# A filter and expert kernel: half of the third batch brought back in column tiles, the second batch's way back drawn into the last 24-point stage

## What is computed

```
out[i] = gate_w[i] * (relu(x[i] @ w1[e]) @ w2[e])
```

## Time and profile before

| what | value |
|---|---|
| runs | 571.74, 576.24, 576.70 us (median 576.24) |
| the profiled execution | 571.98 us, of which the span from the first to the last instruction is 570.1 us |
| mean granted TensorE clock | 0.944 of full speed |
| busy share of the span | TensorE 85%, weight loads 68%, VectorE 39%, ScalarE 37%, GpSimd 38% |
| moved by DMA | 121.22 MB, 213 GB/s over the span |

### The profile page before, as it was taken

How to read it: one execution, slowest core, us unless ns; L and a number is a source line. 1 busy time by engine, 2 the same in 40 slices (tenths; PEclk the granted TensorE clock), 3 DMA queues, 4 the chain that set the end, 5 groups by cost and what they waited for, 6 DMA issues and landing times.

```text
span 570.1 us, 9642 instructions
## 1 busy us (share of the span) xinstructions
PE 483.7 (85%) x3864; PEld 386.9 (68%) x3864; DVE 220.1 (39%) x334; ACT 213.7 (37%) x378; POOL 216.8 (38%) x189
## 2 busy tenths in 40 slices
PE   5457676899989958977981699999999999999995
PEld 2124232355545534667971699999999999999994
DVE  6024132233355769167700453324433244332210
ACT  2202222444525535635110445424454244443320
POOL 7070100000000000484077227765587655876212
PEclk9859998999989988899986799999999999999999
DMA  8899997979677649789721021983119741193001
GB/s 293 304 348 414 411 309 242 324 246 288 209 243 263 214 133 341 275 291 407 255 83 55 18 93 43 384 296 113 46 62 388 279 129 37 57 389 129 28 21 43
DMA packets 63973, 121.22 MB, mean 213 GB/s; under 512 B 7696, under 2 KB 35120, under 8 KB 63920
## 3 DMA queue, kind: packets, MB, share of 16 engines
q1 hardware_dynamic: 37824, 66.17, 33.4%
q10 hardware_dynamic: 16304, 29.01, 14.3%
q0 software_dynamic: 9792, 25.34, 12.4%
HBM read 60.69 MB, written 59.81 MB: 211 GB/s over the span
## 4 chain that ended last, share of the span: by engine, by line
PE 73%; DMA 8%; issue 5%; DVE 5%; ACT 4%; ACTq 3%; SPq 0%; POOLq 0%; POOL 0%; DVEq 0%
PE back L1050 22%; PE wide L1036 12%; PE bank L1036 12%; PE back L364 7%; PE bank L390 6%; PE wide L351 4%; PE bank L379 3%; DMA v_in<-u_scratch 3%; DMA t_scratch<-t_out 2%; PE bank L403 2%; ACTq L505 2%; DVE pq L599 2%; PE bank L1019 2%; PE bank L417 1%; ACT t_out L498 1%
## 5 line engine op out<-in xcount | busy, mean ns | idle before, releaser
L1050 PE MATMUL back<-w2h,hh 128*128 128x256 f32 x384 | 110.4, 288 | 1.0 <-ACT o_out L823 1.0
L1050 PE MATMUL back<-w2l,hh 128*128 128x256 f32 x384 | 109.3, 285 | 0.0
L1050 PE MATMUL back<-w2h,hl 128*128 128x256 f32 x384 | 109.3, 285 | 0.0
L599 DVE TENSOR_TENSOR pq<-wide,fab 128x1024 f32<-128x1024 f32 x48 | 58.8, 1224 | 118.2 <-PE wide L351 118.2
L865 DVE SCALAR_TENSOR_TENSOR hl<-wide,hh 128x384 fp32r<-128x384 f32 x64 | 34.6, 555 | 133.8 <-ACT hh L814 104.8
L954 POOL DMA_INDIRECT out<-o_out,token x48 | 52.3, 1090 | 82.2 <-ACT o_out L823 72.6
L1050 PEld LDWEIGHTS back<-w2h,hh 128*128 128x128 f32 x384 | 74.3, 194 | 1.2 <-ACT o_out L823 1.2
L1050 PEld LDWEIGHTS back<-w2h,hl 128*128 128x128 f32 x384 | 74.4, 194 | 0.0
L1050 PEld LDWEIGHTS back<-w2l,hh 128*128 128x128 f32 x384 | 74.3, 194 | 0.0
L926 POOL DMA_INDIRECT g_in<-y_rows,token x48 | 51.4, 1072 | 57.2 <-DVE token L737 35.1
L823 ACT ACTIVATE o_out<-back,o_gate 128x256 f32<-128x256 f32 x48 | 22.7, 476 | 103.4 <-PE back L1050 86.5
(11 more groups left out here) (109 smaller groups left out, 802.8 us busy)
## 6 DMA issues: line engine op xcount, KB each, us to landing
out<-zero SPq DMA_DIRECT2D x24, 1024.0 KB
w_raw<-in_w SPq DMA_DIRECT2D x16, 1024.0 KB
u_scratch<-v_out ACTq DMA_DIRECT2D x48, 192.0 KB, 3.6
v_in<-u_scratch SPq DMA_DIRECT2D x36, 256.0 KB, 5.2
y_rows<-y ACTq DMA_DIRECT2D x18, 512.0 KB, 3.8
t_scratch<-t_out ACTq DMA_DIRECT2D x30, 256.0 KB, 6.2
z_in<-t_scratch SPq DMA_DIRECT2D x24, 256.0 KB, 3.8
x_in<-in_x POOLq DMA_DIRECT2D x12, 512.0 KB, 15.3
```

The costliest lines, as they stand in the source:

```text
L599: nc.vector.tensor_tensor(pq[:, n % 3], wide[:, :, 0, :].unsqueeze(2).to_broadcast([P, 2, 2, D]), fab[:, h], ALU.mult).then_inc(m_done, 1)
L1050: mm = nc.tensor.matmul(ps[4 + (b * ST + s) % 2][:, 0:D], hx[:, b % 2, f, s * P:(s + 1) * P], wt[:, k, f, :], start=(f == 0 and m == 0), s ...
```

## The change

Batch 2 is brought back only for the rows of its first half (1536 rows, the first 64 of the 128 positions), and only these are routed. A product of 128 output positions becomes two of 64, side by side on the array's columns, one for each half of the 24 points, so six products replace twelve. They need all rows of the scratch, so the bytes loaded stay the same; they come in three pieces (2, 4 and 6 of 12 points from each half), four DMAs each. Routing of this batch uses other masks and token numbers (`tri_half`, `half_hi`, `half_lo`) and its own table and counts; if the eight lists are not full after it, the second round starts with the whole third batch. The test moves into routing step 29 of the half batch.

In the last 24-point stage the tokens of batch 1 go at three steps per two h, from h = 3 to h = 12; all six of their chunks are loaded at once, into the buffer that held x. Batch 0's table and routing end there too (h = 11), and batch 1's routing steps 0 to 7 run at h = 13 to 15, its rank product right behind the stage. Behind the stage, SP issues expert 0's weights first, then the three pieces. ScalarE casts expert 0's weights before batch 2's token steps and expert 1's w1 after them. GpSimd's difference of expert 0's w2 comes ahead of the gathers. Stages 0 and 1 and the experts keep their order.

```diff
+LAST_FROM = 3
+LAST_EXP = 4
+LAST_RANK = 4
+LAST_TABLE = 10
+NEXT_EXP = 14
+NEXT_TABLE = 2
+LAST_STEPS = [0, 0, 0, 4, 8, 12, 18, 23, 25, 27, 28, 30, 30, 30, 30, 30]
+NEXT_STEPS = [0, 0, 0, 0, 0, 0, 0, 0, 0, 0, 0, 0, 0, 4, 7, 8]
...
+def products(t):
+    return N2 // 4 if t == HALF else N2 // 2
...
+def late_tokens(h):
+    n = h - LAST_FROM
+    return range(0) if n < 0 else range((3 * n + 1) // 2, (3 * n + 4) // 2)
...
+        def v_piece(sp, t, k):
+            lo, hi = ((0, 2), (2, 6), (6, 12))[k]
+            to = v_half[k // 2]
+            for a in range(2):
+                for s in range(2):
+                    sp.dma_start(to[a:P:2, s, lo % 6:lo % 6 + hi - lo, :],
+                                 from_u(t, a)[:, HN * s + lo:HN * s + hi, :]).then_inc(v_loaded[k], 16)
...
+                elif ai is not None and g == 0:
+                    v_ready(sp, ai)
+                    sp.wait_ge(a_done, (t + 1) * 12)
+                    sp.nop(nofuse=True)
+                    for c in range(NCH):
+                        v_chunk(sp, ai, c)
...
         def sp_last(sp, t, r):
-            for c in range(3):
-                v_load(sp, t, c)
             sp.wait_ge(bi_done, (t + 1) * NG)
             raw_load(sp, r, 0, 0)
             raw_load(sp, r, 0, 1)
-            for c in range(3, NCH):
-                v_load(sp, t, c)
+            v_ready(sp, t)
+            sp.wait_ge(ya_done, ya_before(t))
+            sp.nop(nofuse=True)
+            if t == HALF:
+                for k in range(3):
+                    v_piece(sp, t, k)
...
             raw_load(sp, r, 1, 0)
             raw_load(sp, r, 1, 1)
...
+            if t == HALF:
+                for s in range(2):
+                    mm = nc.tensor.matmul(ps[i % 2][s * A1:(s + 1) * A1, :], wai[:, 0:A1],
+                                          v_half[i // 3][:, s, 2 * (i % 3):2 * (i % 3) + 2, :], start=True, stop=True)
...
+        def pe_last_stage(pe, t, r, after_another):
+            ai, rt = t - 1, t - 2
+            for h in range(NH):
+                if h == LAST_TABLE + 1:
+                    pe.wait_ge(m_done, t * NH + h)
+                    pe_table(pe, rt, 2)
+                if h == LAST_TABLE + 2:
+                    pe.wait_ge(route_step, rt * ROUTE_STEPS + TABLED)
+                pe_forward(pe, t, r, h)
...
+                if NH + h < AI_FROM + span(rt):
+                    pe_tokens(pe, rt, NH + h - AI_FROM, t + 1, False)
+                for i in late_tokens(h):
+                    pe_tokens(pe, ai, i, t + 1, False, rt if i > LAST_RANK else None)
+                    if i == LAST_RANK:
+                        pe_rank(pe, rt, 7)
+                if h >= 2 and h % 2 == 0:
+                    pe_inverse(pe, t, h // 2 - 1)
+            pe_inverse(pe, t, NG - 1)
+            pe_rank(pe, ai, 7)
...
-        def pe_last(pe, t, before):
-            for i in range(NH - before, AI_SPAN):
-                pe_tokens(pe, t - 1, i, t + 1, False)
+        def pe_last(pe, t):
             pe.wait_ge(v_evac, (t + 1) * NG)
-            pe_table(pe, t - 2, 4)
-            for i in range(AI_SPAN):
-                if i == 0:
-                    pe_rank(pe, t - 1, 4)
-                pe_tokens(pe, t, i, t + 1, True)
-                if i == 6:
+            for i in range(span(t)):
+                pe_tokens(pe, t, i, t + 1, True, t - 1)
+                if i == NEXT_TABLE:
                     pe_table(pe, t - 1, 4)
...
+        def act_last(act, t, r):
+            act_split(act, r, 0, 0, t + 1)
+            act_split(act, r, 0, 1, t + 1)
+            for i in range(span(t)):
                 act_tokens(act, t, i, True)
-                if i == 4:
-                    act_split(act, r, 0, 0, t + 1)
-                if i == 6:
-                    act_split(act, r, 0, 1, t + 1)
-                if i == 10:
-                    act_split(act, r, 1, 0, t + 1)
+            act_split(act, r, 1, 0, t + 1)
...
         def dve_last(dve, t, r):
+            for n in range(NEXT_STEPS[-1], HOT):
+                dve_route(dve, t - 1, n, 7)
             if r == 0:
                 dve.wait_ge(bi_done, (t + 1) * NG)
                 nc.vector.memset(zero[:, :], 0.0).then_inc(zero_set, 1)
-            for n in range(HOT, ROUTE_STEPS):
-                dve_route(dve, t - 2, n, 4)
-            for n in range(HOT):
-                dve_route(dve, t - 1, n, 4)
             low_split(dve, r, 0, 0)
...
                 pool.wait_ge(bi_done, (t + 1) * NG)
+                low_split(pool, r, 0, 1)
                 pool.wait_ge(tokens_set, 3)
                 rows_ready(pool, t)
                 pool_gather(pool, r, 0)
-                low_split(pool, r, 0, 1)
                 pool_gather(pool, r, 1)
```

More of the change, by code:

```diff
@@ L63, with batch_of, ya_before, span @@
 STEPS_BY = [0, 0, 0, 3, 6, 8, 10, 12, 14, 16, 19, 22, 24, 26, 27, 28]
+def batch_of(t):
+    return t if t < FIRST else t - 1
+def products(t):
+    return N2 // 4 if t == HALF else N2 // 2
+def ya_before(t):
+    return sum(products(k) for k in range(t))
+def span(t):
+    return products(t) + 3
+def gates_before(t):
+    return 16 * sum(2 if k == HALF else 1 for k in range(t))
+def late_tokens(h):
+    n = h - LAST_FROM
+    return range(0) if n < 0 else range((3 * n + 1) // 2, (3 * n + 4) // 2)
 def spread_rows():
@@ L317, in sp_stage @@
                     z_load(sp, t + 1, n - NG)
-                if ai is not None:
+                if ai is not None and more:
                     if g == 0:
@@ L1105, in stages @@
         def stages(first, last, stage):
-            stage(first, first + 1, 8 if first == 0 else 0, None, None, None, None)
-            stage(first + 1, first + 2, 0, first, AI_FROM, None, None)
-            for t in range(first + 2, last):
-                stage(t, t + 1 if t + 1 < last else None, 0, t - 1, AI_FROM if t + 1 < last else AI_EARLY, AI_FROM, t - 2)
+            stage(first, first + 1, None, None)
+            stage(first + 1, first + 2, first, None)
+            for t in range(first + 2, last - 1):
+                stage(t, t + 1, t - 1, t - 2)
         @block.sync
@@ L1122, in run @@
                     z_load(sp, first, g)
-                stages(first, last, lambda t, a, a_from, ai, ai_from, before, rt: sp_stage(sp, t, ai, a is not None))
+                stages(first, last, lambda t, a, ai, rt: sp_stage(sp, t, ai, True))
+                sp_stage(sp, last - 1, last - 2, False)
                 sp_last(sp, last - 1, r)
@@ L1220, in run, with stage @@
                 load_tables(pool, 3)
-                def stage(t, a, a_from, ai, ai_from, before, rt):
-                    if a is not None and a + 1 < last:
+                def stage(t, a, ai, rt):
+                    if a + 1 < last:
                         for c in range(NCH):
```

362 lines of the change are left out of this document (233 added, 129 removed).

## The result

The changed kernel takes 588.57 us, median of 4 runs (587.59 to 590.48), beside 574.16 for the kernel before in the same session (571.74 to 576.7): ratio 1.0277, 95% interval 1.023 to 1.0323. It is slower; 571.4 was forecast, and the time lies above the range. The profiled execution took 587.59 us, with a span of 585.8.

The account below looks back on a forecast made before the run. TensorE was taken to bound the last 24-point stage and the end, a chain of waits the part between. Stage +6.1, behind it −7.7, DMA row +1.0: −0.6 against 571.98, giving 571.4 us; range 559 to 583.

Parts of the forecast that it names:

- so I charge 1 us: First block: GpSimd's twelve indirect DMAs in a row, 15.7 us, reach into it and cost 1 us.
- T: End of the last inverse of the last 24-point stage; times behind the stage are counted from it.
- some T + 21: Behind the stage: when GpSimd's run of twelve indirect DMAs was expected to begin.
- Rival (c): First block: the twelve DMAs in a row delay ScalarE's copies of first up products; 8 us more, 579.4; chance 0.21.
- from the stage's end to the first block: Behind the last 24-point stage: 34.5 us instead of 42.2, so 7.7 us shorter.
- SP's wait for the last stores of u costs nothing: Ahead of the pieces' loads: the wait lies under expert 0's weights, which need 7 of 17.5 us; priced at nothing.
- no table: Behind the last piece: batch 1's table, 1.2 us before, no longer counted in the 9.5 us of token steps.
- the stage's end: Last 24-point stage: ends at some 212.1 us, 6.1 later than 205.95; bounds 3.8 and 8.6 later.
- three multiplies 3.7, steps 3.0: Last 24-point stage, h = 13 to 15: VectorE's multiplies and batch 1's routing steps, within 9.4 us to the stage's end.
- Rival (b): Stretch 291.0 to 324.6: if late completions there need the zeros, up to 16 us go, 555; chance 0.07.
- Rival (a): Stage ends only 3.8 later, pieces load at 381 GB/s, the 1.0 doesn't show: 7.6 us faster, 564.4; chance 0.28.
- (d): Half batch leaves an expert under 768 rows; a second round runs, costing more than 248 us; chance 0.01.

Follow-up runs that it names:

- f2: Changed kernel, batch 1's routing steps 0 to 7 behind the stage and GpSimd's difference between the gathers, against the kernel before, chip 2: 576.0 us, ratio 1.005.
- a1: The changed kernel itself, run again beside the kernel before on chip 3: ratio 1.0085.
- e5: Kernel before with its row of 24 indirect DMAs cut by waits for up products, against the kernel before, chip 3: ratio 1.0111.
- g1: Kernel before with its row of 24 indirect DMAs cut another way, block 4's gather earlier, against the kernel before, chip 8: ratio 1.0009.
- f1: Changed kernel with batch 1's routing steps 0 to 7 behind the last 24-point stage, against the kernel before, chip 2: 588.37 us, ratio 1.0266.
- e1: Changed kernel with GpSimd held behind its first three gathers until the half batch's last raw, against the kernel before, chip 3: ratio 1.0019.
- e2: Changed kernel with SyncE's stores of zeros held until the half batch's last raw, against the kernel before, chip 3: ratio 1.0016.
- f4: Changed kernel, batch 1's routing steps 0 to 7 behind the stage and stores of zeros held, against the kernel before, chip 2: 584.95 us, ratio 1.0238.
- e2b: Changed kernel with the stores of zeros held, run a second time against the kernel before, chip 3: ratio 1.0044.

## Why the prediction was wrong, point by point

The step that failed is the charge for the twelve indirect DMAs in a row: **"so I charge 1 us"**. The mechanism was seen, in the earlier trace rows, and the row was named as new; its price and its place were wrong. I reckoned that it "reach[es] into the first block", where TensorE has four banks to go ahead in. It ran beside the last token steps, from T + 26 to T + 41.6, where each step waits for the one before and no bank helps. It also began 5 us later than "some T + 21": the table that it needs, counted as read "at about T + 18", stands behind the second half product, which waits for its load. On chip 2 the runs give 9.0 us for the row alone and 12.4 with the zeros beside it, and nothing that they resolve on chip 3. It speaks for the place that in f2 nine of the twelve DMAs follow one another beside the first block (246.85 to 259.46), where ScalarE waits for TensorE 2.53 us at most. Rival (c), slower with a chance of 0.21, was this case with another place ("ScalarE's copies of the first up products") and a wait of 8 us; "against it that the run is half as long" weighed its length and not what stands beside it.

The second failed step is "from the stage's end to the first block", forecast 7.7 us shorter. Without late completions it is T + 38.9 in f2, 3.3 shorter than the 42.2 of the earlier trace rows, and T + 39.5 in a1, where e5 and g1, which until then are the kernel before, have T + 39.0 and T + 41.1. The tokens end at T + 34.2 in f2, not at T + 29.0. Three terms were wrong. **"SP's wait for the last stores of u costs nothing"**: those stores take 7.02 us beside the weights, and 2.71 without them, so the pieces were issued at T + 8.6, and the last one lands at T + 22.6 (234.90), not at T + 19.5, and behind the bound of T + 21.4. Issuing the weights first was thus paid by the stores, which I had looked at only as something to hide. Next, the token steps were counted from the last piece (9.5 us), but nothing waits for it: in f2 it lands at 234.40, and the product that needs it starts at 236.17. The second piece holds the tokens. It lands at T + 18.4, and five of the six products stand behind it, 15.6 us (230.18 to 245.8). Last, "no table" was wrong, and so was one price for every half product. f2's chain behind the second piece, with products (L506), turns (L524) and batch 1's table (L581), and the granted clock there, columns as in the earlier trace rows:

```profile
230.18 1.97 PE bank L506 x4
232.16 1.05 PE bank L524 x4
233.20 1.43 PE bank L506 x4
234.63 0.59 PE back L524 x4
235.22 1.02 PE back L581 x24
236.24 1.01 PE bank L506 x4
```

```profile
230.00:234.00 4.00, 3.82 (x10) 1.30 (x12) 0.00 (x0) 1.17 (x2) 0.00 (x0) 0.50 1.06 353
```

The table takes 1.02 us of them. The first two of these products and the turn between them run at the lower clock, 1.2 GHz (0.50), after a stretch in which TensorE was busy for 0.61 of 13 us (212 to 225) and 1.98 of 5 us (225 to 230). Against 1.01 and 0.59 they cost 1.8 us more. The kernel before paid a part of this too: its clock was 0.70 from 228 to 232.

With the stage 6.3 later (212.28 − 205.95), 3.3 won behind it (f2) and 12.0 for the row with the zeros beside it (T + 50.9 against f2's T + 38.9), the sum is 15.0, the 15.0 by which the first block moved. It closes by construction, as the 12.0 is what is left; f1 and f2 give 12.4 for it.

Right: the stage's end, 212.28 for 212.1. That it fits to 0.2 us is luck, as T lies between 209.6 and 214.4 in five executions of the same code on chip 3. In three of them (a1, e1, e2) the last inverse takes 3.2 to 3.4 us instead of 1.95, in a1 at a granted clock of 0.55 (209.9 to 213.4), after a stretch in which TensorE was busy for 3.73 of 6.90 us. And "three multiplies 3.7, steps 3.0" had the wrong split: in the changed kernel the forwards of h = 13 to 15 start at 203.44, 205.49 and 207.93, in f1, with no steps, at 204.08, 206.13 and 208.31. The pace is the hand-over between the two engines; the steps cost some 0.6 (from the first of these forwards to T it is 8.8 and 8.2). Right, too: the half product. At the full clock its records are 1.08 us and the next row starts 1.01 later, so its two matmuls run side by side and not one after the other; the 1.98 of the first two is the clock. The Trainium skill, "TensorEngine Tiling (Array Packing)", "Key Properties", says that a change of tiling mode drains TensorE. The trace agrees with a little of it: a turn behind a half product takes 0.59 to the next row where the earlier trace rows has 0.53 ahead of logits, and a half product 1.01 where a whole one had 0.96, some 0.1 us a step.

The cast of w1 of expert 1 on the path, 1.91, stands in the chain as priced, and the row of 24 and the stretch behind the first block are as they were (322.6 against 321.9). Rival (b), that the stretch of 291 to 324.6 needs the zeros, is out: their issue ended at 262.06 instead of 264.30, while the stretch moved 15 us later, and it stayed. Rival (a)'s faster loads did not come: the last piece landed at T + 22.6 and not at T + 15.8. No second round ran, so (d) is out.

## What to carry to other kernels

A row of instructions that is harmless where the engines run ahead of one another can cost more than half its length (9.0 of 15.4 us in f4, on one of four chips) where a chain of small dependent steps runs beside it: before moving anything out of the middle of such a row, look at what the other engines do then, and leave a pause in it. An edit of one line can move more than it names, as the cut of the row moved the zeros: look at every engine's queue before two runs are said to differ in one thing. A wait that "lies under" a transfer is itself a transfer that shares the engines with it: price it beside the load, not alone. And measure on more than one chip before a loss or a gain of a few per cent is put down to the code.

## What the runs showed of the hardware that was not expected

- Chips differ, in one thing that can be seen: on chip 2 and in the first measurement, ScalarE got TensorE's completions up to 13 us late while GpSimd issued indirect DMAs in a row (1.0 us each with 0.3 between). On chips 3 and 9 it got them at once beside the same row of twelve, and on chip 8 beside a row of fifteen. The kernel before takes 572.7 us on the one and 554 to 556 on the others. What makes the difference no run here shows. Only chip 3 was measured twice, so chip and session aren't told apart.
- It is TensorE's signal that comes late. In the changed kernel its semaphore updates come later and later behind its instructions, from 0.24 to 10.31 us, while ScalarE's own signal went through at once beside the same row (its copy at 253.07 ends at 253.34, and TensorE starts on it at 253.39). The ends of matmuls in the profile are modelled, so whether TensorE finishes late or only its signal comes late stays open.
- A difference on VectorE took 6.06 us, where the earlier trace rows have 2.28, because GpSimd's of the same shape began 0.76 us ahead of it, VectorE's line first:

```profile
225.04 6.06 DVE L969 TENSOR_TENSOR w1l<-w_raw,w1h 128x2048 fp32r<-128x2048 f32 x1
```

```profile
224.28 4.67 POOL L969 TENSOR_TENSOR w2l<-w_raw,w2h 128x2048 fp32r<-128x2048 f32 x1 [11.69 <-ACT w2h L961]
```

  GpSimd's ends at 228.95; 2.28 behind that is 231.23, and VectorE's ends at 231.10: it waited for the whole of the other. The Trainium skill, "SBUF — State Buffer", "SBUF: two separate sides", says so: the pair of ports that the two engines share is locked for a whole instruction and not divided. The trace agrees. Here it lay under a wait and cost nothing.
- ScalarE's issue of the last two row stores takes 2.14 us in a1, beside the zeros, and 1.10 in e2 and 1.67 in e2b on the same chip, where the zeros are held; in the first measurement it took 2.94.
